# Twelve weight pieces of the first layer split on VectorE instead of GpSimd, the first group's low parts on GpSimd, the table of decays moved, the weights asked for behind the rows

## The reference, cut to what matters

```
attention (per batch, head; 768 steps):
  m_new = max(f + m, i);  C = exp(f+m-m_new)*C + exp(i-m_new) * v k^T;  n likewise with k
  y = sigmoid(o) * (C q) / max(|n q|, 1)
x = y as 1536 rows of 320
layer 1:  h = x @ w_in (320x2048);  g = h if h>=1, 0 if h<=-1, else (h+1)^2/4;  x = g @ w_out (2048x320)
layer 2:  P = Sinkhorn(exp(x @ w_gate)) over 8 experts;  out = sum_e P[:,e] * (relu(x @ w1[e]) @ w2[e])
```

## Time and profile before

| | |
|---|---|
| runs shown, median of 3 | 956.74 us (956.52 to 957.06) |
| the profiled execution, its own time | 956.86 us |
| its span in the trace | 955.1 us |
| PE busy | 947.2 us, 99% of the span |
| DVE, ACT, POOL busy | 379.5, 254.8, 225.3 us |
| mean granted clock of TensorE | 0.994 of full speed |

### The profile page before, as it was taken

The page is one execution under the profiler, slowest core; times in us unless marked ns, Lnnn a source line. Parts: engine busy times, 40 slices in busy tenths (PEclk is TensorE's granted clock), DMA queues, the critical chain, the costliest instruction groups (busy, mean ns, idle before and its releaser), DMA issues.

```text
span 955.1 us, 16999 instructions
## 1 busy us (share of the span) xinstructions
PE 947.2 (99%) x7157; PEld 866.3 (91%) x7157; DVE 379.5 (40%) x704; ACT 254.8 (27%) x498; POOL 225.3 (24%) x209
## 2 busy tenths in 40 slices
PE   9999999999999999999999999999999999999998
PEld 7799999999988989889999888999888999988998
DVE  6787665556432654333222222222222222222222
ACT  3544433335432212221212221122222112221111
POOL 5974555441210111110111110111110111110000
PEclk8999999999999999999999999999999999999999
DMA  8723224101611111000110001011001101100000
GB/s 297 228 68 110 76 67 123 43 2 42 154 32 45 42 43 42 27 16 29 42 42 29 28 15 42 29 42 42 29 12 31 42 28 43 41 2 1 29 28 28
DMA packets 29381, 50.38 MB, mean 53 GB/s; under 512 B 2416, under 2 KB 16864, under 8 KB 28928
## 3 DMA queue, kind: packets, MB, share of 16 engines
q1 hardware_dynamic: 28160, 43.59, 15.4%
q10 hardware_dynamic: 1152, 5.77, 1.6%
HBM read 44.15 MB, written 2.05 MB: 48 GB/s over the span
## 4 chain that ended last, share of the span: by engine, by line
PE 93%; DVE 3%; DMA 2%; ACT 1%; SPq 0%; issue 0%; DVEq 0%; ACTq 0%
PE bank L1344 35%; PE bank L1357 35%; PE bank L1232 9%; PE bank L1242 5%; PE bank L1246 3%; PE bank L1157 2%; DMA qk_s<-qk 1%; DMA factors<-dec 1%; PE bank L1130 1%; PE bank L1092 1%; PE bank L1151 1%; DVE ht_lo L940 1%; PE bank L1268 1%; PE bank L1147 0%; DVE h_lo L1033 0%
## 5 line engine op out<-in xcount | busy, mean ns | idle before, releaser
L1357 PE MATMUL bank<-e_hi,h_hi 128*128 128x320 f32 x768 | 241.0, 314 | 0.0
L1357 PE MATMUL bank<-e_lo,h_hi 128*128 128x320 f32 x768 | 237.4, 309 | 0.0
L1357 PE MATMUL bank<-e_hi,h_lo 128*128 128x320 f32 x768 | 237.3, 309 | 0.0
L568 ACT ACTIVATE h_hi<-bank 128x512 fp32r<-128x512 f32 x192 | 104.4, 595 | 469.8 <-PE bank L1344 469.8
L597 POOL TENSOR_TENSOR e_lo<-raw,e_hi 128x640 fp32r<-128x640 f32 x64 | 100.1, 1577 | 545.5 <-ACT e_hi L415 545.5
L1033 DVE SCALAR_TENSOR_TENSOR h_lo<-bank,h_hi 128x512 fp32r<-128x512 f32 x192 | 123.8, 686 | 244.8 <-ACT h_hi L568 244.8
L1357 PEld LDWEIGHTS bank<-e_hi,h_hi 128*128 128x128 f32 x768 | 144.2, 188 | 8.1 <-issue 8.0
L1357 PEld LDWEIGHTS bank<-e_lo,h_hi 128*128 128x128 f32 x768 | 144.3, 188 | 0.0
L1357 PEld LDWEIGHTS bank<-e_hi,h_lo 128*128 128x128 f32 x768 | 144.2, 188 | 0.0
L1050 DVE SCALAR_TENSOR_TENSOR acc<-bank,prob,acc 128x320 f32<-128x320 f32 x84 | 46.3, 551 | 216.5 <-PE bank L1357 216.5
L1344 PE MATMUL bank<-xt_hi,e_hi 64*128 64x512 f32 x576 | 118.0, 401 | 0.1
(11 more groups left out here) (134 smaller groups left out, 1139.1 us busy)
## 6 DMA issues: line engine op xcount, KB each, us to landing
raw<-pieces SPq DMA_DIRECT2D x64, 320.0 KB, 2.9
rw<-rows SPq DMA_DIRECT2D x12, 480.0 KB, 6.8
qk_s<-qk SPq DMA_DIRECT2D x12, 416.0 KB
fb<-factors SPq DMA_DIRECT2D x9, 512.0 KB, 5.9
m_raw<-up_down ACTq DMA_DIRECT2D x2, 1440.0 KB, 9.9
result<-acc SPq DMA_DIRECT2D x12, 160.0 KB, 1.8
decb<-factors SPq DMA_DIRECT2D x18, 80.0 KB
m_raw<-up_down ACTq DMA_DIRECT2D x1, 1152.0 KB, 11.2
```

Of the source, the lines that this page charges most:

```text
L568: nc.scalar.activation(h_hi[:, f, :], ps_h2[f % 4][:, :], ACT.Relu).then_inc(hi2, 1)
L1357: ins = mm(ps_out2[t % 2][:, 0:DM], h[:, f, t * P:(t + 1) * P], w[:, col:col + DM], start=(f == 0 and i == 0), stop=(f == FT2 - 1 and i == 2))
```

## The change: what it does

**Who splits.** POOL splits only pieces 0 to 3 (`EARLY_PIECES`): piece 0 before the first two `over_den`, pieces 1 and 2 after the third, piece 3 in step 1 of group 0. The other twelve are split by DVE in `late_piece`, in the steps that `LATE` names, at the end of a step; a second semaphore `m_split_late` counts them, and `piece_done` chooses the semaphore for those who wait. ACT makes a late piece's high part one step ahead (`LATE.get(f + 1)`). In return DVE no longer makes the low parts `ht_lo` of group 0; POOL does, as in groups 1 and 2.

**Where `dec` lies.** Beside `ig` in the region of `m_hi`, now from piece 10 on (`TABLES`); DVE's wait for `dec_stored` is gone, and ACT waits for it inside piece 10, between the copy and the masked copy.

**When the weights are asked for.** Each of the four transfers is issued later in ACT's list: the first after `turn_factors(1)` instead of before it, the second after `gates_exp(2)` instead of before it, the third after two output gates. Pieces and copies in ACT's list change places with it.

**Order and filling.** DVE's `outputs(0, 0)` goes behind `chunk_decays(2)`. PE gets two more `keep_busy` products before `spread_decays` and two new ones behind `weights(0, 2)`.

```diff
@@ -39,12 +39,12 @@
 PARTS = ((0, P), (P, 2 * P), (2 * P, S))
-EARLY = 6
 SLOTS = 2
 RESTS = 8
-TABLES = 12
+TABLES = 10
+EARLY_PIECES = 4
 LOADS = (0, 2, 6, 11, FT1)
-LATE = {2: (6, 7), 3: (8,), 4: (9,), 7: (10, 11), 8: (12,), 9: (13,), 12: (14,), 13: (15,)}
+LATE = {3: (4, 5), 4: (6,), 5: (7,), 6: (8,), 8: (9, 10), 9: (11,), 10: (12,), 11: (13,), 12: (14,), 13: (15,)}
 FREE = 5
@@ -105,7 +105,6 @@
     first_f = sb("first_f", [GH, S])
-    dec = sb("dec", [GH, S])
     assert mark[0] <= after_hidden
@@ -145,6 +144,7 @@
     mx = sb("mx", [GH, S + 1])
+    dec = sb("dec", [GH, S])
     dlast = sb("dlast", [GH, C, GH])
@@ -213,6 +213,7 @@
     m_split = mk("m_split")
+    m_split_late = mk("m_split_late")
     piece_in = [mk(f"piece_in{i}") for i in range(SLOTS)]
@@ -307,6 +308,13 @@
+    def piece_done(engine, q):
+
+        if q < EARLY_PIECES:
+            engine.wait_ge(m_split, q + 1)
+        else:
+            engine.wait_ge(m_split_late, q - EARLY_PIECES + 1)
+
     block = nc.Block()
@@ -392,7 +400,7 @@
-            sp.wait_ge(m_split, FT1)
+            piece_done(sp, FT1 - 1)
             for q in range(NP2 - SLOTS):
@@ -430,7 +438,9 @@
                 if q >= RESTS:
-                    act.wait_ge(m_split, q - RESTS + 1)
+                    piece_done(act, q - RESTS)
+                if q == TABLES:
+                    act.wait_ge(dec_stored, 32)
                 nc.scalar.activation(st_hi[:, q % RESTS, :], m_st_raw[:, q, :], ACT.Identity, scale=mask_up).then_inc(m_hi_ready, 1)
@@ -483,30 +493,28 @@
             gates_exp(1)
+            turn_factors(1)
             load_weights(0)
-            turn_factors(1)
+            gates_exp(2)
             load_weights(1)
-            gates_exp(2)
-            load_weights(2)
             first_state(0, ps_o_of[0])
             output_gate(0, 1)
+            load_weights(2)
+            mlp_piece(0)
             first_state(1, ps_o_of[1])
-            mlp_piece(0)
             output_gate(0, 2)
+            mlp_piece(1)
             load_weights(3)
-            mlp_piece(1)
+            mlp_piece(2)
             twice(0, 0)
-            mlp_piece(2)
             twice(1, 1)
             mlp_piece(3)
-            mlp_piece(4)
-            mlp_piece(5)
@@ -545,7 +553,7 @@
             def mlp_piece_at(f):
-                for q in LATE.get(f, ()):
+                for q in LATE.get(f + 1, ()):
                     mlp_piece(q)
@@ -686,17 +694,14 @@
             decayed_values(0, 2, False)
+            mlp_piece(0)
             over_den(0, 0)
             over_den(0, 1)
-            mlp_piece(0)
             pool.wait_ge(dE_ready, 1)
             mlp_piece(2)
-            mlp_piece(3)
-            mlp_piece(4)
-            mlp_piece(5)
@@ -724,11 +729,11 @@
-            def mlp_piece_at(f):
-                for q in LATE.get(f, ()):
-                    mlp_piece(q)
-
-            attention(1, mlp_piece_at, False)
+            def last_early_piece(f):
+                if f == 1:
+                    mlp_piece(EARLY_PIECES - 1)
+
+            attention(1, last_early_piece, True)
             for ga in range(2, G):
@@ -896,10 +901,10 @@
             denominators(0, 1, ps_o_of[1])
-            outputs(0, 0, ps_o_of[0])
             decay_columns(1, ps_dE)
             chunk_decays(2)
+            outputs(0, 0, ps_o_of[0])
             outputs(0, 1, ps_o_of[1])
@@ -910,12 +915,18 @@
             dve.wait_ge(f_stored, 32)
-            dve.wait_ge(dec_stored, 32)
                     turn_lo(xm_hi, g * GT + t, banks[t], g * GN + t * P, xm_ready)
+
+            def late_piece(q):
+
+                dve.wait_ge(m_hi_ready, q + 1)
+                cols, rows_ = slice(q * PM, (q + 1) * PM), slice(q * PS, (q + 1) * PS)
+                tt(m_lo[:, cols], m_raw[:, q, :], m_hi[:, cols].bitcast(f32), ALU.subtract)
+                tt(m_st[:, rows_], m_st_raw[:, q, :], st_hi[:, q % RESTS, :].bitcast(f32), ALU.subtract).then_inc(m_split_late, 1)
@@ -956,6 +967,8 @@
                         decays(g + 1, i, r)
+                    for q in LATE.get(f, ()) if first else ():
+                        late_piece(q)
                     if next_too and f >= FT1:
@@ -963,7 +976,7 @@
-            mlp(0, True, True, True, True)
+            mlp(0, True, True, False, True)
             for g in range(1, G - 1):
@@ -1197,9 +1210,10 @@
             pe.wait_ge(wt_ready, 4)
-            keep_busy(ps_o_of[1], 2)
+            keep_busy(ps_o_of[1], 4)
             spread_decays()
             weights(0, 2)
+            keep_busy(ps_o_of[1], 2)
             heads(0, 1, ps_o_of[1], past=False)
@@ -1276,7 +1290,7 @@
                     if first and f < FT1:
-                        pe.wait_ge(m_split, f + 1)
+                        piece_done(pe, f)
                     if f < FT1:
                         if f == 0:
```

## The result

| | before | changed |
|---|---|---|
| median | 956.89 us (956.52 to 958.85, 5 runs) | 962.48 us (961.63 to 963.02, 5 runs) |
| ratio | | 1.0055, 95% interval 1.0040 to 1.0069 |
| profiled execution, its span | 956.86, 955.1 us | 962.48, 960.7 us |

The account below looks back on a forecast made before the run. TensorE bounds the kernel, busy 947.2 of 955.1 us; only prologue and group 0 could pay. Gains of 2.9 + 0.3 + 0.6 + 0.2 make 4.0 us, giving 952.7 us; range 950.2 to 956.6.

Parts of the forecast that it names:

- The clock stays at 1.00 with the four products: Prologue: four extra `keep_busy`, costing 1.04 us, keep PE's clock at 1.00; 4.58 us saved, 3.5 net.
- the rival that it falls anyway: Prologue: the clock drops despite the extra products, total 956.8 us; chance 0.18.
- The sequence: Group 0, first product to step 3: GpSimd late for piece 3, 9.0 us instead of 9.34, a gain of 0.3.
- The first product of layer 1: End of the prologue: starts near 29.3 us instead of 32.17, a gain of 2.9.
- 0.2 us of gain: Prologue: the first unit's rows land earlier, worth some 0.2 us.
- the 0.9 us to be given back: End of the prologue: DVE comes late to the third unit's denominators, losing 0.9 of the 3.8 us gained.
- DMA runs full until about 34 us in any case, so the bytes only change their order: Prologue transfers: three of four weights transfers move one place back; unit 2's rows would land near 15 us, not 18.49.
- the 0.2 us: Start of layer 1: queries of unit 3 land before PE wants them, a gain of 0.2 us.
- so they fit: Group 0 on DVE: twelve pieces at 1.03 us, 12.4 us in all, fit into 23.0 us of idle time.
- DVE becomes the bound: Group 0: pieces at 2.8 us each make PE wait, total 960.4 us, slower; chance 0.08.
- 0.6 had been forecast as gain: Group 0 from step 3 on: half of its 1.24 us excess over group 1 is gained back, 0.6 us.
- from the rest: Sum in the rival on DVE: 3.9 us gained elsewhere, set against group 0 lasting 7.5 us more.

Follow-up runs that it names:

- experiment 8: The kernel of experiment 7 without the four extra `keep_busy` products: 962.08 us, ratio 1.0051 to the kernel before.
- experiment 4: The changed kernel with the four weights transfers back at their old places in ACT's list: 961.66 us, ratio 1.0032 to the kernel before.
- experiment 7: The changed kernel with the third weights transfer behind `twice(0, 0)` and the fourth in step 1 of group 0: 956.14 us, ratio 0.9988 to the kernel before.
- experiment 5: The changed kernel with the first layer's weights laid out piece by piece, packets at most 2304 bytes: 959.51 us, ratio 1.0005 to the kernel before.
- experiment 6: The changed kernel with only the fourth weights transfer moved, to step 1 of group 0: 955.77 us, ratio 0.9976 to the kernel before.
- experiment 3: The kernel before with the split changed (twelve pieces on DVE); transfers and fill as before, GpSimd's prologue order as changed: 960.76 us, ratio 1.0020.
- experiment 2: The changed kernel with GpSimd splitting all sixteen pieces again, `ht_lo` of group 0 on DVE: 957.72 us, ratio 0.9996 to the kernel before.
- experiment 10: The changed kernel with DVE's late piece moved from behind the scan to before the maximum: 960.33 us, ratio 1.0017 to the kernel before.
- experiment 12: The kernel of experiment 9 with piece 3 also split by DVE, in step 1: 952.59 us, ratio 0.9937 to the kernel before.
- experiment 9: The kernel of experiment 7 with DVE's late piece moved from behind the scan to before the maximum: 952.70 us, ratio 0.9944 to the kernel before.

## Why the prediction was wrong, point by point

**Right.** The clock stays at 1.00 with the four products; experiment 8 shows it, at a price of 5.9 us where it doesn't, and the rival that it falls anyway is out. The third unit's rows come earlier: 16.99 in place of 18.49, later than the 15 forecast, but needed (experiment 4). The sequence gave 9.0 us from first product to step 3 with GpSimd late there, and with the queries in time it is 9.07, with a wait of 1.25 us for piece 3 (experiment 7).

**Right by luck.** The first product of layer 1, forecast near 29.3, starts at 29.20. But `heads(0, 2)` was to end 3.8 us earlier, near 24.8, and ended at 25.7, 3.0 us earlier. PE was already 0.7 us behind at the first unit's set (12.89 in place of 12.20), having waited 0.45 us for the first queries, where the prediction gave it 0.2 us of gain:

```profile
7.24 1.16 PE L1143 MATMUL bank<-qk_s 40*128 40x128 f32 x16 [0.45 <-DMA qk_s<-qk]
...
12.89 1.98 PE L1170 MATMUL bank<-vi,at 128*128 128x42 f32 x16
...
23.76 1.91 PE L1170 MATMUL bank<-vi,at 128*128 128x42 f32 x16
```

And the 0.9 us to be given back behind it was not: from the end of the heads to the first product it is 3.5 us in both traces. The two errors of 0.9 us cancel.

**The first step that failed:** "DMA runs full until about 34 us in any case, so the bytes only change their order", and with it the 0.2 us "for the queries of unit 3, which now land before PE wants them". They landed at 35.2, against 34.1 before. The prediction reckoned with an even share between the queues, and looked at the rows of unit 2 alone. Experiment 5 and its counts show packets in its place: SP's 512-byte packets pass one for one with ACT's of up to 11520 bytes, so nothing behind `fb` moves until the weights are through, near 30 us. Experiments 6 and 7 show that it is the fourth transfer that must move. The gain of 2.97 us in the prologue became a wait of 4.39 and then the lower clock: together +4.79. The warning stood in the trace of before, in the row at 34.11.

**The second:** twelve pieces against DVE's idle 23.0 us of group 1, "so they fit". The total did fit, and DVE was never full. What counts is the length of the chain in a step: clamp 0.5, wait for the square 0.66, maximum 0.55, scan 1.2, piece 1.7 to 2.3, next clamp. In steps 5 and 6 that is 4.5 and 5.0 us, where PE's steps 6 and 7 take 2.8 and 2.9, so that piece 8 comes 1.64 us late. The prediction even named steps 5, 6 and 8, yet priced them from a mean. The mean of a piece was 1.58 us, above the 1.03 taken and under the 1.9 at which the rival "DVE becomes the bound" was to begin; it began earlier, since the chain in a step counts and not the total. That rival was the right one in kind, with a chance of 0.08 and a condition on the wrong quantity. The pieces cost 2.7 us against the kernel before (55.44, or 55.46 in experiment 3, against 52.78), 4.0 where the clock falls as well (56.77), and 3.8 against GpSimd's splitting in the same prologue (51.66, experiment 2); 0.6 had been forecast as gain. In experiments 10 and 12, with the piece at the other place, the stretch is 52.45 and 52.51 us.

**Two slips in the prediction's sums.** The rival on DVE sets 3.9 us "from the rest" against its 7.5; without the 0.6 that it denies the rest is 3.4, so it stands for 960.9 us. And by its own terms the range begins at 949.9 rather than 950.2. Neither bears on the result.

**The rule on the shared port.** The Trainium skill's page "SBUF — State Buffer", section "Who interferes with whom", was read as a wait of one GpSimd instruction at most. In the changed kernel an `m_st`, 0.28 us when free, took 1.79 at 68.37, while GpSimd did two instructions in a row (67.73 to 70.0):

```profile
68.37 1.79 DVE L929 TENSOR_TENSOR m_st<-m_st_raw,st_hi 128x128 fp32r<-128x128 f32 x1
```

```profile
67.73 1.33 POOL L655 TENSOR_TENSOR st_d<-st,dE 104x336 f32<-104x336 f32 x1
69.02 0.99 POOL L605 TENSOR_TENSOR ht_lo<-gact,ht_hi 128x384 fp32r<-128x384 f32 x1
```

A run of GpSimd's instructions without a gap holds DVE until about its end, as the 5.44 us of the earlier trace rows had suggested.

## What to carry to other kernels

Before pricing a faster stretch, follow the chain past its end: list what the next steps wait for, with the time at which each lands now, because the gain can't be larger than the slack of the nearest (here -0.30 us). Work fits into an engine's idle time only where the idle time lies: put it beside a wait that is there anyway (here between the clamp and the maximum, experiment 9), and compare the longest chain within one step with the step, not totals with totals. And read a transfer's landing with the sizes of the packets that share the DMA engines with it.

## What the runs showed of the hardware that was not expected

- Two DMA queues share the engines by packets: 637 packets of 512 bytes beside 536 of 6380 on average, 33 KB against 342 KB per us (changed kernel, 20 to 30 us). A table of 512 KB took 16.1 us beside the large packets, 10.9 beside smaller ones (experiment 5) and 6.3 where the other queue's weights had landed at 19.3 and 21.4, between its issue at 16.7 and its landing at 23.0 (experiment 7).
- Issuing a transfer can hold the engine that issues it: 5.89 us on ACT in experiment 5, where the same issue took 0.48 in the changed kernel, and with it ACT's next copy; 6.50 us for two issues on SP, 1.13 before.
- A wait of 0.43 us can be followed by 3.4 us of TensorE at the 1.2 GHz level (changed kernel at 70.21), while the wait of 1.64 us at step 8 of experiment 7 left it at 2.4 GHz. Eight profiles have the wait of 0.41 to 0.43 us at step 9; in three of them the clock fell there (changed kernel, experiments 4 and 6), in five not. So a wait can cost more than itself, and in some executions only.
- The clock also fell and stayed low for 13.7 us with TensorE busy throughout (experiment 8), and four more products held it up. The spread of the kernel before, 954.2 to 962.8 us on one chip, goes with its mean clock, 0.998 to 0.988. What exactly decides the fall stays open.
